# One block instead of two, w_out fetched first, and per-head state matmuls in a linear attention and two-layer expert kernel

## The reference

```
for t in range(S):
    cur = einsum('bhd,bhe->bhde', u * k[t], v[t])
    y[t] = einsum('bhd,bhde->bhe', r[t], state + cur)
    state = w[t][..., None] * state + einsum('bhd,bhe->bhde', k[t], v[t])
```

## Time and profile before

| what | value |
|---|---|
| median of 3 runs (lowest, highest) | 1072.85 us (1072.76, 1073.62) |
| the profiled execution, its own time | 1071.09 us |
| its span, first to last instruction | 1069.4 us |
| granted TensorE clock, mean | 0.993 |
| TensorE busy (weight loads) | 1019.0 us, 95% (966.7 us, 90%) |
| VectorE, ScalarE, GpSimd busy | 714.7, 591.8, 219.5 us |
| DMA moved, mean rate | 166.37 MB, 156 GB/s |

### The profile page before, as it was taken

How to read it: one execution, slowest core, us unless ns; L and a number is a source line. 1 busy time by engine, 2 the same in 40 slices (tenths; PEclk the granted TensorE clock), 3 DMA queues, 4 the chain that set the end, 5 groups by cost and what they waited for, 6 DMA issues and landing times.

```text
span 1069.4 us, 19880 instructions
## 1 busy us (share of the span) xinstructions
PE 1019.0 (95%) x7471; PEld 966.7 (90%) x7471; DVE 714.7 (67%) x1342; ACT 591.8 (55%) x1125; POOL 219.5 (21%) x208
## 2 busy tenths in 40 slices
PE   4999999999999999999999899999999999999995
PEld 4766699999899998999998899999999999999995
DVE  4678667787787787745667658575665857566570
ACT  3556355655465555533554547565665756566571
POOL 0000000101101110111114423324324332422421
PEclk9899999999999999999999999999999999999998
DMA  9788643558236741020467889788887978889851
GB/s 223 181 182 171 153 67 71 43 96 87 42 55 65 104 68 38 27 71 7 145 147 139 219 235 269 217 246 260 214 283 220 271 214 243 257 219 283 221 156 15
DMA packets 190723, 166.37 MB, mean 156 GB/s; under 512 B 118098, under 2 KB 174292, under 8 KB 190628
## 3 DMA queue, kind: packets, MB, share of 16 engines
q1 hardware_dynamic: 177652, 144.79, 53.4%
q0 software_dynamic: 12976, 20.32, 9.8%
HBM read 141.21 MB, written 25.22 MB: 156 GB/s over the span
## 4 chain that ended last, share of the span: by engine, by line
PE 80%; ACT 2%; DMA 2%; issue 1%; POOL 1%; DVE 1%; another core or an unknown queue 0%; POOLq 0%; DVEq 0%; ACTq 0%
PE pp L1192 18%; PE bank L1176 18%; PE bank L772 17%; PE fx L788 9%; PE yu L1235 3%; PE tr L167 2%; PE pp L182 2%; PE yu L223 2%; PE tr L1157 2%; PE yu L1217 1%; PE fx L1217 1%; PE yu L201 1%; PE yu L218 1%; DMA slot_entry<-entry,slot_i 1%; DMA xr<-ffn_out,who 1%
## 5 line engine op out<-in xcount | busy, mean ns | idle before, releaser
L772 PE MATMUL bank<-xh,w12h 128*128 128x256 f32 x576 | 166.9, 290 | 3.9 <-DVE ab_all L850 3.9
L772 PE MATMUL bank<-xl,w12h 128*128 128x256 f32 x576 | 162.8, 283 | 0.0
L772 PE MATMUL bank<-xh,w12l 128*128 128x256 f32 x576 | 162.7, 283 | 0.0
L1090 POOL DMA_INDIRECT result<-x2s,who x55 | 93.3, 1696 | 282.4 <-ACT x2s L1309 269.9
L1296 DVE SCALAR_TENSOR_TENSOR abl<-bank,abh 128x512 fp32r<-128x512 f32 x96 | 66.2, 691 | 110.6 <-ACT abh L1291 77.3
L947 POOL DMA_INDIRECT slot_entry<-entry,slot_i x48 | 49.9, 1040 | 381.2 <-DVE token_f L938 369.9
L772 PEld LDWEIGHTS bank<-xh,w12h 128*128 128x128 f32 x576 | 110.1, 191 | 6.6 <-DVE ab_all L850 4.9
L772 PEld LDWEIGHTS bank<-xl,w12h 128*128 128x128 f32 x576 | 110.2, 191 | 0.0
L772 PEld LDWEIGHTS bank<-xh,w12l 128*128 128x128 f32 x576 | 110.1, 191 | 0.0
L1176 PE MATMUL bank<-xh,set_up_h 128*128 128x256 f32 x384 | 109.2, 284 | 0.2 <-DVE abl L1296 0.2
L1176 PE MATMUL bank<-xh,set_up_l 128*128 128x256 f32 x384 | 108.6, 283 | 0.0
(11 more groups left out here) (235 smaller groups left out, 2792.1 us busy)
## 6 DMA issues: line engine op xcount, KB each, us to landing
up_raw<-in_moe_w SPq DMA_DIRECT2D x93, 512.0 KB
down_raw<-in_moe_w SPq DMA_DIRECT2D x124, 384.0 KB
padded<-in_w SPq DMA_DIRECT2D x32, 144.0 KB
padded<-in_k SPq DMA_DIRECT2D x32, 144.0 KB
padded<-in_r SPq DMA_DIRECT2D x32, 144.0 KB, 4.4
vs<-in_v SPq DMA_DIRECT2D x32, 144.0 KB, 3.2
attention_out<-yt SPq DMA_DIRECT2D x64, 72.0 KB
result<-zeros SPq DMA_DIRECT2D x3, 1536.0 KB
```

Source lines behind the costliest of these rows:

```text
L772: last = nc.tensor.matmul(bank[f % 2][:, m * TG:(m + 1) * TG], wp[:, m, kk, f * P:(f + 1) * P], xp[:, kk, :], start=(n == 0), stop=(n == 3 ...
L1090: nc.gpsimd.indirect_dma_start(out, bass.IndirectOffsetOnAxis(who[v % 4][:, s, 0:1], 0), yo[v % 2][:, s, 0:DM], None, bounds_check=N - 1, ...
```

## The change

The edit has these parts.

1. **Transfers at the start.** After `w` of pair 0 SyncE starts w_out in two halves, each with a semaphore of its own, then `k`, w3 block 0, `r`, `u`, `v`, and so on. The two gate matrices are started from ScalarE's queue. "wo_turn" goes through the first half of w_out and then the second, and waits for each half alone; "wo_gates" waits for the gates. `first_slots` gives another order of the first pair's steps.
2. **Transfers of later pairs.** One input at a time: `k` and `r` of the pair after next at "score" 0 and 1, each behind a wait on the scores, and `w` of the next pair at "in" 1, behind a wait on the transposes.
3. **State by head.** "state" computes only each head's own 48 x 48 part: two matmuls of 64 stationary columns and 48 moving columns for each border in place of one; VectorE copies 240 columns in place of masking 480, its four steps and ScalarE's five work on 48 columns in place of 96; the state part of "out" is two matmuls of 48 rows and 64 stationary columns in place of one of 128 x 128. `head_block` goes. `state` and `ruk` get two buffers each, and two waits loosen by a pair.
4. **One block.** The bodies of both blocks become functions, and each engine runs its first and then its second in one block. What the end of the first block had ordered is now ordered by waits: on `w12l_ready`, `wa_full`, `wb_free`, `wal_ready`, `pads_stored`, `row_cleared`.
5. **Zero fills.** The three fills of a third of the output become twelve of a twelfth, one behind the first store of each pair in the dense stage; GpSimd's first addition waits for all of them. The load of token group 2 moves ahead to a "down" step.

```diff
         xh, xl = sb("xh", [P, KD, TG], f32r), sb("xl", [P, KD, TG], f32r)
...
-        head_block = asb("head_block", [P, 2, D])
...
-        ruk = asb("ruk", [P, NC, 2, D])
...
         kend_t = asb("kend_t", [P, NC - 1, P])
         att = asb("att", [P, 2, 2, 3, C])
...
-        state = asb("state", [P, NC - 1, 2, HB])
+        added = [asb(f"added{i}", [P, NC - 1, D]) for i in range(2)]
...
-        def sp_inputs_load(sp, b, q):
+        def sp_input_load(sp, b, q, n):
             g, i = HP * b + q, q % 2
             need(sp, tr_full, 4 * (g - 2) + 3)
             need(sp, ruk_ready, g - 1)
-            for n, x in enumerate((w, k, r)):
-                for h in range(2):
-                    sp.dma_start(padded[i][:, n, :, h, 0:D],
-                                 x[bass.ds(b, 1), 2 * q + h, :, :].rearrange("o (c p) d -> p (o c) d", p=C)
-                                 ).then_inc(loaded[n][i], 16)
+            for h in range(2):
+                sp.dma_start(padded[i][:, n, :, h, 0:D],
+                             (w, k, r)[n][bass.ds(b, 1), 2 * q + h, :, :].rearrange("o (c p) d -> p (o c) d", p=C)
+                             ).then_inc(loaded[n][i], 16)
...
             for c in range(NC - 1):
-                last = nc.tensor.matmul(yu[:, c * 96:(c + 1) * 96], kend_t[:, c, :],
-                                        vs[q % 2][:, c, :, 0:D], start=True, stop=True)
+                for h in range(2):
+                    rows = slice(h * HB, (h + 1) * HB)
+                    last = nc.tensor.matmul(yu[rows, c * D:(c + 1) * D], kend_t[:, c, rows],
+                                            vs[q % 2][:, c, h, 0:D], start=True, stop=True)
...
-                    nc.tensor.matmul(yu[:, n * C:(n + 1) * C], state[:, c - 1, :, :].rearrange("p h x -> p (h x)"),
-                                     rdec[q % 2][:, c * C:(c + 1) * C], start=(c == (1, 3)[half]), stop=False, skip_group_check=True)
+                    for h in range(2):
+                        rows = slice(h * HB, h * HB + D)
+                        nc.tensor.matmul(yu[h * HB:(h + 1) * HB, n * C:(n + 1) * C], state[q % 2][rows, c - 1, :],
+                                         rdec[q % 2][rows, c * C:(c + 1) * C], start=(c == (1, 3)[half]), stop=False,
+                                         skip_group_check=True)
...
-                nc.vector.tensor_tensor(ruk[:, :, :, :], padded[i][:, 1, :, :, 0:D], padded[i][:, 2, :, :, 0:D],
+                need(dve, diag_ready, g - 1)
+                nc.vector.tensor_tensor(ruk[q % 2][:, :, :, :], padded[i][:, 1, :, :, 0:D], padded[i][:, 2, :, :, 0:D],
...
-            hb = head_block[:, :, :].rearrange("p h d -> p (h d)")
-            nc.vector.tensor_tensor(added[q % 2][:, :, :], yu[:, 0:480].rearrange("p (c x) -> p c x", c=NC - 1),
-                                    bass.AP(hb.tensor, hb.offset, [hb.ap[0], [0, NC - 1], [1, 96]]),
-                                    ALU.mult).then_inc(yu_free, 1)
+            nc.vector.tensor_copy(added[q % 2][:, :, :], yu[:, 0:(NC - 1) * D].rearrange("p (c x) -> p c x", c=NC - 1)
...
             g = HP * b + q
-            need(act, yu_full, 3 * g)
...
-                nc.scalar.activation(state[:, c, :, 0:D], added[q % 2][:, c, :].rearrange("p (h d) -> p h d", h=2), ACT.Copy,
+                nc.scalar.activation(state[q % 2][:, c, 0:D], added[q % 2][:, c, :], ACT.Copy,
                                      scale=decay[q % 2][:, c, C:C + 1]).then_inc(state_ready, 1)
...
-            return [[("in", 0, 0)], [("in", 0, 1), ("derive", 0, 0), ("diag", 0, 0)], [("in", 0, 2), ("derive", 0, 1), ("diag", 0, 1)],
-                    [("derive", 0, 2), ("diag", 0, 2)], [("derive", 0, 3), ("spread", 0, 0)],
-                    [("derive", 0, 4), ("derive", 0, 5), ("spread", 0, 1)], []]
+            return [[("in", 0, 0)], [("derive", 0, 0)], [("in", 0, 1), ("derive", 0, 1)],
+                    [("in", 0, 2), ("derive", 0, 2), ("diag", 0, 0)], [("derive", 0, 3), ("diag", 0, 1)],
+                    [("diag", 0, 2), ("derive", 0, 4), ("spread", 0, 0)], [("derive", 0, 5), ("spread", 0, 1)]]
...
+
+            g = HP * b + q
             if step == "out":
                 sp_attention_store(sp, b, q, n)
                 if n == 1 and later(b, q + 2):
                     sp_values_load(sp, *later(b, q + 2))
-            elif step == "score" and n == 1 and later(b, q + 2):
-                sp_inputs_load(sp, *later(b, q + 2))
+            elif step == "score" and later(b, q + 2):
+                sp.wait_ge(pp_full, 2 * g + n + 1)
+                sp_input_load(sp, *later(b, q + 2), n + 1)
+            elif step == "in" and n == 1 and later(b, q + 1):
+                sp.wait_ge(tr_full, 4 * g + 2)
+                sp_input_load(sp, *later(b, q + 1), 0)
...
+            def first_sp(sp):
...
+                sp_input_load(sp, 0, 0, 0)
+                for part in range(2):
+                    sp.dma_start(wo[:, 4 * part:4 * part + 4, 0:DM],
+                                 w_out[part * F1 // 2:(part + 1) * F1 // 2, :].rearrange("(m p) d -> p m d", p=P)
+                                 ).then_inc(wo_loaded[part], 16)
+                sp_input_load(sp, 0, 0, 1)
+                load_w3(0)
+                sp_input_load(sp, 0, 0, 2)
+                sp.dma_start(u_all[:, :, :, :].rearrange("p q h d -> p (q h d)"),
+                             bass.AP(u.tensor, u.offset, [[0, P], [1, H * D]])).then_inc(small_loaded, 16)
+                sp_values_load(sp, 0, 0)
+                load_w12(0)
+                for n in range(3):
+                    sp_input_load(sp, 0, 1, n)
+                load_w3(1)
+                sp_values_load(sp, 0, 1)
+                load_w12(1)
+                for step, q, n in order:
+                    if step == "w3_turn" and n == 1 and q + 2 < KF:
+                        load_w3(q + 2)
+                    elif step == "w3_mm" and n == 3 and q + 2 < 6:
+                        load_w12(q + 2)
...
+            def first_act(act):
+                for part, x in enumerate((w_gate, w_noise)):
+                    nc.scalar.dma_start(gates[:, :, part * E:(part + 1) * E], x.rearrange("(m p) e -> p m e", p=P)
+                                        ).then_inc(gates_loaded, 16)
...
+                    if step == "wo_turn":
+                        part, kk = divmod(q, KD)
+                        if kk == 0:
+                            pe.wait_ge(wo_loaded[part], 16)
...
+                            pe.wait_ge(wb_free, 6)
+                            pe.wait_ge(gates_loaded, 32)
...
+            def sp_clear(sp, part):
+
+                rows = N // CLEARS
+                sp.dma_start(out[part * rows:(part + 1) * rows, :].rearrange("(p n) (h d) -> p (n h) d", p=P, h=2),
+                             zeros[:, :].rearrange("p (o d) -> p o d", o=1).broadcast_to([P, 2 * rows // P, DM // 2])
+                             ).then_inc(zeros_stored, 16)
...
+                    if i == 0:
+                        pe.wait_ge(wb_free, 6 + 2 * KF)
+                if f == 1 and i == 0:
+                    pe.wait_ge(wal_ready, KF)
                 need(pe, ab_free, KF * i + f - 1)
...
+                if i == 0:
+                    pool.wait_ge(pads_stored, 16)
...
+                        pool.wait_ge(zeros_stored, 16 * CLEARS)
                     stands_alone(pool, pool_added)
...
+            def rest_sp(sp):
+                sp.wait_ge(w12l_ready, 2 * KD)
+                for q in range(1, NG):
+                    sp_group_load(sp, 0, q)
+                sp.wait_ge(wa_full, KF)
+                sp.dma_start(noise_all[:, :, :], noise.rearrange("(n p) e -> p n e", p=P)).then_inc(noise_loaded, 16)
+                for b in range(B - 1):
+                    for step, q, n in both:
+                        if step == "down" and n == 5:
+                            sp_group_store(sp, b, q)
+                        elif (step, q, n) == ("down", NG - 1, 3):
+                            sp.wait_ge(fx_free, fx_down(b, q, 0) + 1)
+                            sp_group_load(sp, b + 1, NG - 1)
+                        elif step == "score" or step == "in":
+                            if later(b + 1, q):
+                                sp_attention(sp, later(b + 1, q)[0], step, later(b + 1, q)[1], n)
+                        elif step == "out":
+                            sp_attention(sp, b + 1, step, q, n)
+                            if n == 0:
+                                sp_clear(sp, HP * b + q)
+                            if q == HP - 1:
+                                sp_group_load(sp, b + 1, n)
+                sp_group_store(sp, B - 1, 0)
+                sp_rows(sp, 0)
...
+                pool_scatter(pool, B - 2, NG - 1)
+                pool.wait_ge(row_cleared, 16)
```

More of the change, by code:

```diff
@@ new lines, in rest_dve, with group @@
+            def rest_dve(dve):
+                def group(b, step, q, n):
+                    bb, q = of_group(b, q)
```

(36 more changed lines are left out.)

632 lines of the change are left out of this document (276 added, 356 removed).

## The result

The changed kernel takes 1058.48 us (median of four runs, 1056.99 to 1061.47) beside 1073.23 us for the kernel before in the same comparison: ratio 0.9871, interval 0.985 to 0.9892, so 14.75 us faster. The forecast was 9.2 us, its range 1055 to 1072. The profiled execution takes 1058.37 us, its span is 1056.5 us, and its mean granted clock is 0.991.

What follows compares the result with a forecast made beforehand. TensorE was taken to set the pace, so edits pay only by filling its gaps or removing its work. Terms -7.0 - 1.8 - 2.5 + 2.1 = -9.2 us took the median from 1072.85 to 1063.7 us, range 1055 to 1072.

Steps and rivals of the forecast that it cites:

- The start: First transfers and TensorE's early idle gap: w_out sooner, scores of pair 0 at about 22.2 us, -7.0 us.
- The seam: Between the two blocks: TensorE's idle 2.58 us goes, a wait for the token split remains, -1.8 us.
- The state chain: VectorE's smaller state copy and scale-and-adds shorten TensorE's waits for ScalarE's `wt` copy, -2.5 us.
- The state matmuls: State and output matmuls on TensorE, twice as many but smaller, at 67 ns an instruction: +2.1 us over 16 pairs.
- Rival B: State matmuls: weight loads of halves overlap too, so they cost -10.7 us, total 1050.9 us; chance 0.16.
- The queues: Later pair loads and zero fills moved on SyncE's queue stay hidden, 0 us.
- Rival D: Output state matmuls: halves serialise in one PSUM bank, +15.2 us instead of +2.1, total 1076.8 us; chance 0.09.
- Rival C: Start: transfers behind w_out set the pace to about 30 us, gain only -2 us, total 1068.7 us; chance 0.12.
- E: Whole kernel: the edits don't bite, another order of waits eats the gaps, about 1072 us; chance 0.07.

Runs made afterwards that it cites:

- e1: The kernel before with only the new start (transfer order, w_out in halves, gates on ScalarE's queue, first pair's order): ratio 0.9922, 8.4 us of 1075.59.
- e3: The changed kernel with its two halves in two blocks again, nothing else moved: ratio 0.9896.
- e10: The kernel before with the state-by-head part alone (smaller matmuls, copy for mask, two buffers each): ratio 0.994, 6.5 us of 1075.67.
- e11: The changed kernel, unmodified, run a third time: ratio 0.9812.
- e5: The changed kernel with nine forms of matmul, 20 each, twice over, added behind all its work: 30 to 116 ns an instruction.
- e8: The changed kernel with the twelve zero fills back in the weight stage, three behind each pair's first output store: ratio 0.9851, median 1063.95 us.
- e9: The changed kernel, unmodified, run again: ratio 0.9891, profiled execution 1074.1 us.
- third group: Runs on one chip beside the kernel before: added matmul forms, state-by-head alone, the changed kernel again and with two steps swapped: ratios 0.9812 to 0.994 where given.
- second group: Runs on one chip beside the kernel before: the changed kernel again, and with copy as addition, with steps also swapped, or with early fills: ratios 0.9851 to 0.9903.

## Why the prediction was right, and what in it was not

The mechanism is the forecast one in the main: TensorE sets the pace, and the change fills its start, its seam and its waits. One term had the wrong sign. The terms:

1. **The start, forecast -7.0, read 8.0.** The first w_out transpose was put at 6.8 us and is at 7.21, the gates at about 15 (15.68), the scores at 22.2 (22.21); the lead is still 8.7 in the second pair. The 1 us taken off for the later stream did not appear. e1 gives 8.4 us, though its interval (5.1 to 11.7) does not tell 7 from 8.
2. **The seam, forecast -1.8, read 1.8.** The lead is 7.64 us at the last w3 matmul and 9.44 at the first dense one. e3 puts it at 2.2, or 1.8 without its half-clock part. The wait on VectorE's split came nearly as forecast, 0.60 us for 0.8.
3. **The state chain, forecast -2.5.** The instructions shrank as forecast. In the profile of the changed kernel the waits for `wt` hardly did, 6.0 us, where 3 to 4 were expected; in e10 they are 3.3 and in e11 2.1. So the term is right for the work; the late starts (2 x 1.3 us, and TensorE's 1.4 behind each, 2.8 of the 6.0) hid it in the profiled execution.
4. **The state matmuls, forecast +2.1, read -2.3.** This is the step that failed, in size and in sign, by 4.4 of the 5.6 us between forecast gain and result. "At 67 ns: L201 1.34 us" priced halves of 48 moving columns with L223, whose halves have 128. In e5 one half with 128 moving takes 111.5 ns and its load of 64 columns 60.5, so L223's 67 was its stream. With 48 moving columns the load is the longer, and two halves side by side take 30. The old product took 120 ns since full-size loads of 128 columns need 113 whatever moves: halving the width halves that. Rival B said this of L201, 40 ns; it is 36. L217 gains nothing, and there both the forecast and B compared runs with their ends to rates without: twice as many instructions at half the time (55 ns without the ends of its short runs, (0.80 - 0.58) / 4 instructions) are the same work as before (0.11 us an instruction, (0.76 - 0.54) / 2). B's 54 ns was right for that rate, and its gain against "135 ns" was only the old run's ends; 10 instructions took 0.54 + 0.76 = 1.30 us, not 1.35. What no term has is the price of entering the small matmuls, 0.09 to 0.10 us, 32 times: 3 us that the smaller state product has to earn first.
   The Trainium skill, page TensorE: Matmul & The Clock Gate, section LDWEIGHTS (loading the stationary operand), puts a load at its columns divided by 1.2 in ns; worked out from that, as an estimate, 107 for 128 columns and 53 for 64. In e5 the forms that wait for their load take 113 to 116 and 60.5, so the trace agrees to within 14%.
5. **The queues, forecast 0.** e8's steps, within 0.3 us, confirm it for the fills at TensorE; the one-by-one loads were not tested alone.

With -2.3 for term 4 the forecast's own sum would have been -7.0 - 1.8 - 2.5 - 2.3 = -13.6 us, 1059.3; measured 1058.48. That it comes so near is in part luck: in the profile the half-clock stretch and the late starts take away 4.5 us, while the visits, of which no term speaks, give 2.

**Rival D**, that L217's halves serialise at 108 ns in one bank, is refuted: 67 to 73 ns in the kernel, 56 alone, against 54.5 with two banks. The rule that stood beside it, in the Trainium skill, page TensorEngine Tiling (Array Packing), section Gotcha 1: PSUM Pressure, does not hold for two row halves that write different partitions of a bank: the measurement decides. **Rival C**, that the queue takes the start back, is refuted by the scores at 22.21 and 23.01 us and by the lead that is left at the last w3 matmul, 7.6 and in e1 6.6 us, and **E** by the total. **Rival B** has the load right, but its term of -10.7 us is refuted by the 2.3 read.

What stays open: what delays VectorE's copy in some executions, and why a half-clock stretch comes at 68 us in some. The three ratios of the changed kernel, 0.9812 to 0.9891, span 8.5 us. Late starts stand in the profiles of the two higher ones and not in that of the lowest. In the first profile they cost about 2.8 us and the stretch at 68 us 1.7; in e9's, two more half-clock stretches cost 9.4. The clock also goes with the scatter inside one group: the fastest of the 17 executions of the kernel before in the third group, 1071.58 us, has a mean granted clock of 0.991, the slowest, 1081.98 us, one of 0.982. The rest of the spread, and why the groups differ, I did not trace.

## What to carry to other kernels

To price a matmul of a shape that the trace lacks, work out its load (stationary columns) and its stream (moving columns) apart and take the longer, then halve it if two halves of the array alternate; the nearest row is only near if the same one of the two binds it. Here small products per head cost less than one wide product with a mask (0.72 us for 1.20 on TensorE), and less behind it too, while a product whose stream stayed as long (L217) gained nothing and paid 0.27 us a pair for its entries and ends. So count the short runs too. And measure a part by itself on the kernel before, not only by taking it out of the kernel after: in a single profile, a half-clock stretch and two late starts (4.5 us) were as large as the part (4.2).

## What the runs showed of the hardware that was not expected

**The clock fell under full load.** Two windows of e5, both inside uninterrupted matmuls:

```profile
1060.00:1061.00 1.00, 1.00 (x11) 1.00 (x10) 0.00 (x0) 0.00 (x0) 0.00 (x0) 1.00 0.00 0
...
1063.00:1064.00 1.00, 1.00 (x9) 0.89 (x10) 0.00 (x0) 0.00 (x0) 0.00 (x0) 0.50 0.00 0
```

TensorE had been busy without a gap since 1048.78 us, its last 3.6 us with one half of 48 rows by 64 columns alone, when the granted clock went to 0.50 at 1061.4. The next form took 4.46 us for its 40 instructions instead of 2.33. The second time through the same sequence it did not fall. In the kernels, a stretch that begins inside the gate matmuls of 16 columns came in all profiles, of before and after; in the three of the changed kernel it ended at 26.5, 26.9 and 31.4 us. What brings it about is not shown.

**Row halves share a bank almost for free**: 56 ns against 54.5 in two banks.

**VectorE starts late now and then**: 1.2 to 2.1 us, at the state copy of the second pair of batches 2 and 3, in five profiled executions of the changed kernel and variants with one block, and not in five others of the same kind. All profiles of the second group have them, and none of the first and third. No engine or transfer in the trace explains it; GpSimd's scatter runs beside that copy in e11 too (268.16 to 269.12 us), where the copy starts on time at 269.01.
